# The logits of head u+4 move to the end of unit u, and two first loads of w3 go by ScalarE's queue: an attention and two-layer-MLP kernel on one core

## What is computed

```python
q_assign, k_assign = argmax over 16 centroids of (q_n . c_n), (k_n . c_n)    # B=2, H=8, S=768, D=64
scores = where(q_assign == k_assign, q @ k.T / 8, -1e9)
attn_out = softmax(scores) @ v                       # heads side by side: x is (1536, 512)
h  = ((x @ w1) * (x @ w2)) @ w3 @ w_out              # 512 -> 1024 -> 1024 -> 512
g  = h2 * clip(h2 + 3, 0, 6) / 6, h2 = h @ w_in      # 512 -> 2048
out = g @ w_out2                                     # 2048 -> 512
```

## Time and profile before

| | |
|---|---|
| median of 3 runs | 714.13 us |
| the profiled execution: time, span from first to last instruction | 715.35 us, 713.5 us |
| TensorE (PE) busy | 705.0 us, 99% |
| VectorE (DVE) / ScalarE (ACT) / GpSimd (POOL) busy | 70% / 55% / 63% |
| TensorE's granted clock | 1.000 |
| DMA queues: SP's / ScalarE's | 64.81 MB, 32.2% / 2.93 MB, 1.4% of 16 engines' span |

### The profile page before, as it was taken

The page is one execution under the profiler, slowest core; times in us unless marked ns, Lnnn a source line. Parts: engine busy times, 40 slices in busy tenths (PEclk is TensorE's granted clock), DMA queues, the critical chain, the costliest instruction groups (busy, mean ns, idle before and its releaser), DMA issues.

```text
span 713.5 us, 11831 instructions
## 1 busy us (share of the span) xinstructions
PE 705.0 (99%) x4017; PEld 607.4 (85%) x4017; DVE 496.1 (70%) x754; ACT 390.9 (55%) x808; POOL 446.5 (63%) x455
## 2 busy tenths in 40 slices
PE   8998999999999999999999999999999999999998
PEld 6787777776767767999999999999988889998886
DVE  6237787877878786677986779888865547874221
ACT  6315565656656575454554445477754447775333
POOL 5953553453354475996969969788557769753221
PEclk9999999999999999999999999999999999999999
DMA  8647765665565413211002110012212233221212
GB/s 294 188 105 201 185 124 133 162 162 139 142 168 125 111 23 71 71 65 55 15 16 86 64 60 1 30 60 89 75 47 73 74 102 120 74 76 60 69 35 90
DMA packets 41772, 68.50 MB, mean 96 GB/s; under 512 B 10224, under 2 KB 17904, under 8 KB 41712
## 3 DMA queue, kind: packets, MB, share of 16 engines
q1 hardware_dynamic: 36048, 64.81, 32.2%
q10 hardware_dynamic: 5664, 2.93, 1.4%
HBM read 44.07 MB, written 3.19 MB: 66 GB/s over the span
## 4 chain that ended last, share of the span: by engine, by line
PE 93%; issue 2%; DVE 2%; ACT 1%; POOL 1%; DMA 1%; SPq 0%; POOLq 0%
PE ps L1377 21%; PE ps L1379 21%; PE ps L1378 21%; PE ps L1503 9%; PE ps L1489 8%; PE ps L1477 5%; PE ps L1479 4%; PE ps L1446 1%; DMA wo_raw<-in_wo 1%; DVE g_lo L1295 1%; ACT probs L799 0%; PE ps L1463 0%; PE ps L1408 0%; PE ps L1411 0%; DVE neg_max L1159 0%
## 5 line engine op out<-in xcount | busy, mean ns | idle before, releaser
L634 POOL TENSOR_TENSOR b_lo<-stage,b_hi 128x512 fp32r<-128x512 f32 x94 | 111.9, 1191 | 101.3 <-ACT b_hi L882 101.1
L1295 DVE TENSOR_TENSOR g_lo<-gate,g_hi 128x384 fp32r<-128x384 f32 x96 | 83.6, 878 | 64.9 <-ACT g_hi L971 64.8
L799 ACT ACTIVATE probs<-ps,neg_max 128x768 f32<-128x768 f32 x96 | 86.8, 904 | 51.4 <-DVE neg_max L1159 50.6
L1159 DVE TENSOR_REDUCE neg_max<-ps 128x1 f32<-128x768 f32 x96 | 91.2, 952 | 25.1 <-PE ps L1479 24.9
L971 ACT CAST g_hi<-gate 128x384 fp32r<-128x384 f32 x96 | 49.2, 514 | 90.4 <-PE ps L1379 90.4
L1489 PE MATMUL ps<-ident,probs 128*128 128x128 f32 x576 | 77.6, 275 | 0.0
L1489 PEld LDWEIGHTS ps<-ident,probs 128*128 128x128 f32 x576 | 66.1, 140 | 13.4 <-ACT probs L799 7.2
L1220 DVE COPY probs_t<-ps 128x512 f32<-128x512 f32 x96 | 63.7, 679 | 17.3 <-PE ps L1489 17.1
L591 POOL TENSOR_TENSOR x_lo<-x_raw,x_hi 128x384 fp32r<-128x384 f32 x15 | 15.2, 1016 | 96.7 <-PE ps L1489 64.4
L1180 DVE TENSOR_TENSOR sum_lo<-sum_raw,sum_hi 128x768 fp32r<-128x768 f32 x64 | 65.2, 1021 | 14.5 <-ACT sum_hi L858 14.3
L1379 PE MATMUL ps<-b_hi,g_lo 128*128 128x512 f32 x192 | 74.8, 389 | 0.0
(11 more groups left out here) (129 smaller groups left out, 1846.7 us busy)
## 6 DMA issues: line engine op xcount, KB each, us to landing
stage<-in_wio SPq DMA_DIRECT2D x64, 256.0 KB, 2.6
qk_ops<-qk_split SPq DMA_DIRECT2D x32, 384.0 KB, 5.8
stage<-in_w SPq DMA_DIRECT2D x46, 256.0 KB, 3.1
qk_raw<-in_qk SPq DMA_DIRECT2D x16, 384.0 KB, 5.2
qk_ops<-qk_split SPq DMA_DIRECT2D x32, 192.0 KB, 5.7
v_raw<-in_v SPq DMA_DIRECT2D x16, 192.0 KB, 2.6
recip_all<-recip_rows SPq DMA_DIRECT2D x32, 96.0 KB, 3.1
out<-out_sb ACTq DMA_DIRECT2D x11, 256.0 KB, 2.2
```

The lines of the kernel that those rows point to most:

```text
L634: nc.gpsimd.tensor_tensor(b_lo[n % 2][:, cols], stage[n % 2][:, cols], b_hi[n % 2][:, cols].bitcast(F32), ALU.subtract).then_inc(s_lo[half ...
L799: nc.scalar.activation(probs[g % PROBS][:].rearrange("p (a b) -> p a b", a=2), scores[g % 2], ACT.Exp, bias=neg_max[:, g:g + 1], scale=1.0 ...
L1159: nc.vector.tensor_reduce(neg_max[:, g:g + 1], scores[g % 2], AX.XY, ALU.max, negate=True).then_inc(s_max, 1)
L1295: nc.vector.tensor_tensor(g_lo[i][:], hidden(q, c, f)[0][:], g_hi[i][:].bitcast(F32), ALU.subtract).then_inc(s_glo, 1)
```

## The change

The last two uses of the ring in unit u (groups 6 and 7) get the logits of head u+4 ahead of them; the logits at the start of a unit go. TensorE and ScalarE follow: `logits(u + 4)` stands between `score(s + 7)` and `transposes(s + 4)`, `rows_of_logits(u + 4)` ahead of `group_copies(s + 4)`. On SP `load_raw(4)` stands ahead of the v tiles, and the loads of w12 behind `load_mask(2)`. In the fold the REST of blocks 0 and 1 is issued by ScalarE behind the Sqrt of the centroid norms, so that on SP wo's tiles 2 and 3 follow tile 1 directly. The identity is multiplied 9 times rather than 8.

```diff
--- before.py
+++ after.py
@@ -66,8 +66,6 @@
     uses = [(use, n) for use in ("logits", "cols", "hot") for n in range(2)] + [("logits", 2), ("cols", 2)]
     for u in range(UNITS + 1):
         s = ST * u
-        if u and head(u + 3):
-            uses.append(("logits", u + 3))
         if u:
             uses += fills(s - 1)
         if u == 0:
@@ -79,7 +77,11 @@
         if head(u + 3):
             uses.append(("cols", u + 3))
         if u < UNITS:
-            uses += fills(s + 2) + fills(s + 3) + fills(s + 4)
+            uses += fills(s + 2) + fills(s + 3)
+        if head(u + 4):
+            uses.append(("logits", u + 4))
+        if u < UNITS:
+            uses += fills(s + 4)
     return uses
 
 
@@ -447,16 +449,11 @@
             def load_piece(n):
                 sp.dma_start(stage[n][:, PIECE], w3[n][:, PIECE]).then_inc(s_piece[n], 16)
 
-            def load_rest(n):
-                sp.dma_start(stage[n][:, REST], w3[n][:, REST]).then_inc(s_stage[0][n], 16)
-
             sp.dma_start(cent_raw[:], cent).then_inc(s_cent, 16)
             load_piece(0)
             load_wo(0)
             load_piece(1)
             load_wo(1)
-            load_rest(0)
-            load_rest(1)
             load_wo(2, 3)
             load_half(0, 1, w3[0])
             load_wo(4)
@@ -508,10 +505,9 @@
             load_raw(3)
             load_mask(0)
             load_mask(1)
+            load_raw(4)
             for n in range(4):
                 load_v(n)
-            load(GATE0, w12[0])
-            load(GATE0 + 1, w12[1])
             def spread_recips(u):
 
                 sp.wait_ge(s_rrow, 16 * (u + 1))
@@ -521,12 +517,15 @@
                                  ).then_inc(s_rall[u % 2], 16)
 
             for n in range(2, HEADS):
-                if n + 2 < HEADS:
+                if n >= 3 and n + 2 < HEADS:
                     load_raw(n + 2)
                 load_ops(n)
                 if n >= 3:
                     spread_recips(n - 3)
                 load_mask(n)
+                if n == 2:
+                    load(GATE0, w12[0])
+                    load(GATE0 + 1, w12[1])
                 if n % 2 == 1 and n >= 5:
                     load_v(n - 1)
                     load_v(n)
@@ -823,6 +822,8 @@
 
             act.wait_ge(s_cent_sq, 1)
             nc.scalar.activation(cs[1][:], cs[0][:], ACT.Sqrt).then_inc(s_sqrt, 1)
+            for n in range(2):
+                act.dma_start(stage[n][:, REST], w3[n][:, REST]).then_inc(s_stage[0][n], 16)
             piece_high(0)
             wo_high(0)
             piece_high(1)
@@ -897,8 +898,6 @@
                 s = ST * u
                 if u < UNITS:
                     exp(s + 1)
-                if u and head(u + 3):
-                    rows_of_logits(u + 3)
                 if u:
                     group_copies(s - 1)
                 mix_high(0, "attention", s)
@@ -932,6 +931,8 @@
                 mix_high(0, "attention", s + 4)
                 if u == UNITS - 1:
                     block_high_next(GATE0 + 1, 0)
+                if head(u + 4):
+                    rows_of_logits(u + 4)
                 group_copies(s + 4)
                 mix_high(0, "attention", s + 5)
                 if u == UNITS - 2:
@@ -1419,7 +1420,7 @@
                         mm.then_inc(s_up, 1)
 
             pe.wait_ge(s_ident, 1)
-            for i in range(8):
+            for i in range(9):
                 nc.tensor.matmul(ps[:, 7, 0:P], ident[:], ident[:], start=True, stop=True)
             for j in range(F1T):
                 first_fold(j)
@@ -1527,8 +1528,6 @@
             fold(7, 3, 6)
             for u in range(UNITS + 1):
                 s = ST * u
-                if u and head(u + 3):
-                    logits(u + 3)
                 if u < UNITS:
                     score(s + 2)
                 if u == 0:
@@ -1560,6 +1559,8 @@
                         p_times_v(u - 1, t)
                 if u < UNITS - 1:
                     score(s + 7)
+                if head(u + 4):
+                    logits(u + 4)
                 transposes(s + 4)
 
             def wide_product(g, k):
```

## The result

The changed kernel takes 716.39 us, the median of 20 runs (713.53 to 720.04); the kernel before, run beside it, 714.53 us (713.14 to 715.89, 20 runs). The ratio is 1.0029, with a 95% interval of 1.0018 to 1.0040: slower, where the prediction had 711.3 us (710.2 to 713.3) and faster. The profiled execution took 717.16 us with a span of 715.3 us, 1.8 us over that of before.

What follows compares the result with a forecast made beforehand. The prediction took TensorE's work to bound the kernel (93% of what ended last). Its terms, 1.8 + 0.2 + 0.8 + 0 = 2.8 us won, gave 711.3 us against the median of before, range 710.2 to 713.3.

Steps and rivals of the forecast that it cites:

- Part 1: End of unit 0: earlier load of head 4 removes the wait at logits(4); 1.8 us won, bounds 1.3 and 1.9.
- free, over 10 us of cover: SP's queue: w12 loads go some 10 us later but are first used in unit 2, so cost nothing.
- part 2: score(15) in unit 2: its weights, loaded 0.36 us late, gain from SP's earlier list; 0.2 us won.
- Part 3: The other eleven logits: entering them from a score saves 0.09 us per unit; 0.8 us won, bounds 0 and 1.2.
- the rule by the number of mode changes: Logits' move: each tiling mode change drains TensorE, their number stays, so the term is 0 and the sum 2.0 us.
- Rival T: Raised with the experiments: the logits' new place costs the time, the start being mostly harmless; no chance given.
- Part 4: Start: RESTs on ScalarE's queue, wo's tile 2 earlier, ninth product; taken 0, bounds 0.5 us won and 0.6 lost.
- Rival A: Start: tile 1 comes 1.1 us late, TensorE idles ahead of feature 1, its clock halves; 716.0 us, chance 0.05.
- B: Most units: a softmax or ring wait replaces the removed one, stalling TensorE some 0.2 us; 714.0 us, chance 0.12.
- D: Unit 0 to 1: head 4 lands late despite earlier issue, logits(4) stalls as before; 713.5 us, chance 0.05.

Runs made afterwards that it cites:

- raw4_alone: The kernel before with only the load of head 4 moved ahead of the v tiles, logits as before: 713.61 us, ratio 0.9992.
- before_again: The kernel before, unchanged, run and profiled a second time: 714.33 us, ratio 0.9997.
- start_undone: The changed kernel with the start put back as before, w12 still behind the masks of head 2: 714.48 us, ratio 1.0002.
- w12_back: The changed kernel with both the start and the w12 loads put back as before: 712.44 us, ratio 0.9980; repeated, 712.61 us, 0.9972.
- start_alone: The kernel before with only the change's start (RESTs on ScalarE's queue, nine identity products): 715.43 us, ratio 1.0024.
- nine_on_w12_back: w12_back plus only the ninth identity product: 712.84 us, ratio 0.9976.
- rests_first: w12_back plus the change's start, but with the RESTs issued as ScalarE's first instructions instead of behind the Sqrt: 713.05 us, ratio 0.9975.
- w12_early: w12_back with the w12 loads ahead of load_mask(0): 712.90 us, 0.9979; second kernel adds RESTs first and nine products: 713.01 us, 0.9980.
- w12_half: w12_back with half of the w12 loads issued behind the masks of head 2: 713.22 us, ratio 0.9998.
- best_try: rests_first with half of the w12 loads issued behind the masks of head 5: 713.09 us, ratio 0.9986.

## Why the prediction was wrong

**Part 1, the size.** The mechanism was right: in the profile pair 1.79 us were won where 1.8 was forecast. But the 1.8 was read from one execution and summed against the medians. raw4_alone, which has that gain alone, is 0.6 us faster by its ratio (0.3 by the medians), and its interval includes 1. I had noted that 8.9 us was the longest landing of its line and did not draw the conclusion that the stall was above its usual size. The profiled execution's own 715.35 against a median of 714.13 would not have told me: before_again was profiled at 715.18 without the stall.

**Parts 1 and 2, the step that failed most.** "free, over 10 us of cover", which put the moved w12 loads at nothing, looked at when w12 is used, not at what it would stand next to. I took part 2 at 0.2 won, bounds 0.36 won and 0.5 lost; it lost 0.6 us in the changed profile, 1.4 in start_undone, and the place of w12 alone is worth 2.0 and 2.6 us by the medians. I had listed the queue behind the moved loads (head 5, 2 us earlier) but left out ScalarE's store, which is in flight beside them (71.26 to 78.45 after the change), and SP's wait for it, ahead of the masks. An earlier head 5 was counted as harmless; it goes out just ahead of the store, and the store was late in four of ten profiles where that was so and w12 was away.

**Part 3 was right.** From the first product with v in unit 3 to that in unit 12 it is 125.54 us before (98.95 to 224.49), 125.57 in raw4_alone and 124.91 in w12_back (96.62 to 221.53): 0.07 per unit against 0.09 forecast, where the rule by the number of mode changes gave 0. By the ratios w12_back is 0.12% ahead of raw4_alone, from which it differs by the place of the logits alone. Rival T is out.

**Part 4, the start, was taken at 0 and costs 1.1 to 1.7 us.** The right row was in hand: 512 KB between two landings, a full queue. But I put the lateness on tile 1 alone and let both RESTs squeeze in ahead. Tile 1 was late, little in the changed kernel (7.14 instead of 6.80), by 1.4 us in start_alone; what feature 2 waited for each time were the RESTs. On the other queue, issued at 3.0, they shared with 1.3 MB that SP had issued or was about to issue and took 6.4 and 6.9 us instead of 3.8. The Trainium skill (DMA: Bandwidth & Descriptors, Queues, rings and completion order) says that the engines take turns between queues. I used that for the loss of tile 1 only, and not for what the RESTs lose when they leave SP's list. Nothing here shows how the turns were shared out.

**Rival A** (the start takes it back, at half the clock) came nearest, at a chance of 0.05, and by another path: it had the gap ahead of feature 1 for tile 1, and it came ahead of feature 2 for the RESTs. Its 716.0 next to the measured 716.39 is luck, since it had the whole rest of the gain in it and nothing for w12. Its price, 4.7 us, was too high: 3.30 in the changed profile, of which the wait gave 1.6 and the clock the rest. The clock falls in some executions only: 7 of the 20 show a mean of 0.998 or less, with a median of 717.58. The other 13 have one of 716.30, still 1.8 over before, so the clock is not the main part of what makes the kernel slower. Rivals B and D did not happen: the logits at their new place never waited for GpSimd, and the ring's waits cost nothing to be seen. (D's price was summed wrongly: the 1.0 us that it keeps gives 713.1, not 713.5. Nothing hangs on it.)

Added up in shares of before, in %: head 4 early -0.08, logits' place -0.12, w12's place +0.22 to +0.41, start +0.16 to +0.24, so +0.18 to +0.45, around the measured +0.29. Each term carries an interval of 0.1 or more to either side.

The best version found is w12_back (0.9980 and 0.9972), with nine_on_w12_back, rests_first and both w12_early kernels (0.9975 to 0.9980) not to be told from it: 0.2 to 0.3% faster than before, some 4 us faster than the change.

## What to carry to other kernels

A moved transfer has two prices: when its own data is needed, and which small transfer it now stands beside or ahead of; look for stores and semaphore chains that cross its new place. A stall that is the difference of a landing and an arrival should be seen in more than one execution before it is summed; here it followed the landing time of one load (8.9 us in one profile, 7.2 and 7.1 in two). Moving a load to another engine's queue takes it out of the order of need; here it cost 1.5 us when issued behind SP's first transfers, and nothing (but won nothing) when issued ahead of them.

## What was not expected of the hardware

The same 3 KB store (its elements of 4 bytes gathered from 128 partitions) landed in 4.2 to 7.7 us at the same place of the program, in part by what was in flight beside it (the table above). Over one execution of the kernel before, its 16 stores of reciprocals landed after 2.7 to 7.7 us.

The start varies by more than 1 us between executions of one and the same order: the high part of wo's tile 2 began at 9.08 before (the tile had landed at 9.05), at 9.54 in before_again and at 11.16 in w12_half. In before_again pairs of matmuls started 0.85 us apart from 7.07 to 9.63, twice the usual 0.46, while the granted clock of that stretch reads 1.00, and the same is seen in best_try from 7.29 to 9.85; in the changed kernel such a pace stands beside 0.59. So the column does not show every slow stretch at the start, and the distances of the matmuls should be read with it.
